# GpSimd's work on the diagonal term, one loop split in two: all r k u products of a group, then its three sums times v

## What is computed

```python
for t in range(S):
    cur = np.einsum('bhd,bhe->bhde', u[None] * kt, vt)
    y[:, :, t] = np.einsum('bhd,bhde->bhe', rt, state + cur)
    state = wt[:, :, :, None] * state + np.einsum('bhd,bhe->bhde', kt, vt)
...
g = np.where(pos, h, np.where(neg, 0.0, (h + beta) ** 2 / (4.0 * beta)))   # h = x @ w_in
x = g @ w_out
...
out = (silu(x @ w_gate) * (x @ w_val)) @ w_out
```

## Time and profile before

| | |
|---|---|
| three runs | 953.28, 955.07, 956.41 us; median 955.07 |
| the profiled execution, its own time | 953.63 us |
| its span, first to last instruction | 951.8 us |
| granted PE clock | 0.999 of full speed |
| busy | PE 98%, DVE 58%, ACT 41%, POOL 18% of the span |

### The profile page before, as it was taken

One profiled execution on the slowest core, in us unless ns is written; L12 is line 12 of the kernel. 1 busy time (PEld: TensorE's weight loads), 2 busy tenths in 40 slices (PEclk: granted clock), 3 DMA queues, 4 the chain that ended last, 5 costly groups with the idle time before them and its releaser, 6 DMA issues.

```text
span 951.8 us, 20721 instructions
## 1 busy us (share of the span) xinstructions
PE 933.3 (98%) x8344; PEld 917.5 (96%) x8344; DVE 548.2 (58%) x975; ACT 392.2 (41%) x827; POOL 173.4 (18%) x155
## 2 busy tenths in 40 slices
PE   6899999999999999999999999999999999999998
PEld 5889999999999999999999999999999999999997
DVE  8998877877777778774444433334343343434333
ACT  5675545455554545535664222222222222222222
POOL 6993220402204022021444100000000000000000
PEclk9999999999999999999999999999999999999999
DMA  9824443344433444212324010010101001010000
GB/s 311 247 83 179 139 135 127 113 148 131 142 123 118 142 134 132 110 58 92 108 84 131 3 51 1 1 51 1 51 0 50 0 0 50 0 50 0 25 1 27
DMA packets 49715, 79.58 MB, mean 84 GB/s; under 512 B 14784, under 2 KB 35648, under 8 KB 49632
## 3 DMA queue, kind: packets, MB, share of 16 engines
q1 hardware_dynamic: 49632, 78.42, 25.2%
HBM read 60.71 MB, written 17.69 MB: 82 GB/s over the span
## 4 chain that ended last, share of the span: by engine, by line
PE 93%; DVE 4%; issue 1%; ACT 0%; DMA 0%; DVEq 0%
PE bank L1438 51%; PE bank L1466 36%; PE bank L1497 2%; PE bank L1528 2%; PE bank L1523 1%; DVE suf L1131 1%; PE bank L1515 1%; DVE k_r_by_channel L1156 0%; DVE k_r_by_channel L1153 0%; DVE att L1198 0%; DVE gate L1280 0%; DVE glo L1273 0%; DMA w_by_channel<-in_w_channel 0%; DVE diag L1161 0%; DVE w_by_channel L1141 0%
## 5 line engine op out<-in xcount | busy, mean ns | idle before, releaser
L970 ACT ACTIVATE ghi<-gate 128x384 fp32r<-128x384 f32 x224 | 117.3, 524 | 207.4 <-DVE gate L1292 95.4
L1273 DVE TENSOR_TENSOR glo<-gate,ghi 128x384 fp32r<-128x384 f32 x224 | 136.6, 610 | 83.6 <-ACT ghi L970 81.8
L1290 DVE TENSOR_TENSOR gate<-bank,gate 128x384 f32<-128x384 f32 x96 | 53.5, 558 | 215.0 <-ACT gate L1091 215.0
L1438 PE MATMUL bank<-xhi,w2gv_ahi 128*128 128x384 f32 x480 | 161.3, 336 | 0.0
L1438 PE MATMUL bank<-xlo,w2gv_ahi 128*128 128x384 f32 x480 | 161.3, 336 | 0.0
L1438 PE MATMUL bank<-xhi,w2gv_alo 128*128 128x384 f32 x480 | 161.3, 336 | 0.0
L1091 ACT ACTIVATE gate<-bank 128x384 f32<-128x384 f32 x96 | 47.2, 492 | 227.7 <-PE bank L1438 227.7
L1466 PE MATMUL bank<-ghi,w1ohi 128*128 128x384 f32 x384 | 132.7, 346 | 0.9 <-DVE glo L1273 0.9
L1438 PE MATMUL bank<-xhi,w1ihi 128*128 128x384 f32 x384 | 129.5, 337 | 1.4 <-issue 0.9
L1438 PE MATMUL bank<-xhi,w1ilo 128*128 128x384 f32 x384 | 129.4, 337 | 0.0
L1466 PE MATMUL bank<-glo,w1ohi 128*128 128x384 f32 x384 | 129.4, 337 | 0.0
(11 more groups left out here) (105 smaller groups left out, 1550.3 us busy)
## 6 DMA issues: line engine op xcount, KB each, us to landing
r_k_v_by_token<-in_rkv_token SPq DMA_DIRECT2D x21, 672.0 KB, 6.1
k_r_by_channel<-in_kr_channel SPq DMA_DIRECT2D x18, 512.0 KB, 4.9
w_by_channel<-in_w_channel SPq DMA_DIRECT2D x24, 226.2 KB, 3.2
k_blocks_out<-k_blocks SPq DMA_DIRECT2D x18, 256.0 KB, 2.1
k_moved<-k_blocks_out SPq DMA_DIRECT2D x72, 64.0 KB, 2.0
x_t<-ring SPq DMA_DIRECT2D x8, 576.0 KB, 3.2
x_raw<-x_t SPq DMA_DIRECT2D x8, 576.0 KB, 4.0
ring<-in_w_out SPq DMA_DIRECT2D x21, 192.0 KB, 2.8
```

The costliest lines, as they stand in the source:

```text
L970: e.activation(ghi[j % 2][:, :], gate[j % 2][:, :], ACT.Copy).then_inc(M["hi", ph], 1)
L1273: e.tensor_tensor(glo[j % 2][:, :], gate[j % 2][:, :], ghi[j % 2][:, :].bitcast(F32), ALU.subtract)\
L1290: e.tensor_tensor(q, hid[j % 2][:, 0:T], q, ALU.mult).then_inc(M["t", 2], 1)
L1438: m = e.matmul(out, w_of(a, k), x_of(b_, k), start=start and i == 0, stop=stop and i == total - 1)
```

## The change

The loop over the windows is run twice for groups 2 to 7: once for the products, and once more for the values. Groups 0 and 1, and all other engines' programs, keep their order; SP's is the same line for line.

```diff
             for g in range(2, NG):
                 for w in range(NW):
                     diag_products(g, w)
+                for w in range(NW):
                     diag_values(g, w)
```

## The result

The changed kernel takes 961.10 us (median of 6 runs, 958.95 to 962.75), the kernel before 955.23 us (6 runs, 953.28 to 956.41). The ratio is 1.0061, 95% interval 1.0047 to 1.0074: 5.9 us slower, 4.5 to 7.1. The forecast was 959.1 us, +4.0.

The account below looks back on a forecast made before the run. PE was taken to bound the kernel; waits of 3.7 us in five groups plus 0.3 in group 0 gave +4.0, 957.6 for the profiled execution, 959.1 as median. Range 957.1 to 962, or 954.3 to 962 including no change.

Parts of the forecast that it names:

- The bound and the question: Whole kernel: PE sets the time, other engines' gains in phase 1 are worth at most 1.9 us; their lead decides losses.
- Where the products land: Group 3's four moved POOL products, 4 us of work, arrive at 262 to 269 us, in slots 11 to 13.
- The walk: Slots 11 to 13: four products successively delay DVE, lo(14) by 2.42 us against a 1.34 us lead; PE waits 1.08 us.
- The rule behind the walk: When POOL and DVE both wait, DVE keeps its turn behind a scan but loses it between ordinary two-operand instructions, costing 0.82 us.
- Step 4: Slot 12, window 2: L851 runs 268.04 to 268.91 us, so L1156 ends at 269.47 instead of 267.05, 2.42 us late.
- The kind of instruction: In slots 11 to 13, two-SBUF-input DVE instructions and SBUF-reading POOL instructions exclude each other; up to 4 us a group.
- the wait of PE: At tile_out(14), PE waits for lo(14): 1.08 us in the walked group, 2.6 us over the other four, together 3.7 us.
- The turn of group 0: Two products land among group 0's scans and delay lo(0) of group 1 by 0.77 us against 0.49 lead; PE waits 0.3.
- The sum: Whole kernel: 3.7 us from five groups plus 0.3 from group 0 gives +4.0 us, 959.1 us after the median adjustment.
- the case of no change: Rival, 33%: DVE keeps its turn in slot 12's scaling, lo(14)'s delay stays under its lead; 955.4 us.
- the added wait bites: Rival, 1%: `tok` lands 15 us later, making the values and L1234 late; five groups at 1 us, 960 us.
- The heavier case: Rival, 6%: every moved product costs DVE the full 0.82 us, adding 9.8 us in all, 964.9 us.

## Why the prediction was right

- *The bound and the question* held: PE sets the time, what DVE won (its wait at L1162) was worth nothing, as the kernel with the later sum shows by itself, and what it lost counted where it passed the lead.
- *Where the products land* held: POOL's first product starts in the scan, its last ends at 272.24 us, slots 11 to 13.
- *The walk* held step by step in group 3: 0.42, 0.35, 0.83 and 0.82 us were forecast for the four records, 0.35, 0.35, 0.82 and 0.82 measured, 2.42 against 2.34 in all. Who went first was as forecast at each of the four steps.
- *The rule behind the walk* is another matter: that DVE keeps its turn behind a scan and loses it between ordinary instructions holds for the pairs that this walk meets, and not in general. The trace of the kernel before had both counterexamples, which the prediction passed over. Behind the scan that ends at 10.29 us POOL's L848, waiting since 9.70, goes first and L1153 takes 1.42 us; behind the ordinary L1156 of the earlier trace rows, which ends at 40.27, DVE's lo goes first with its 0.55 us, though POOL's L851 has waited since 39.80. DVE's timeline, then POOL's:

```profile
9.05 1.24 DVE L1141 TENSOR_TENSOR_SCAN w_by_channel<-w_by_channel,scan_seed 112x516 f32<-112x516 f32 x1
10.20 1.42 DVE L1153 TENSOR_TENSOR k_r_by_channel<-k_r_by_channel,suf 112x512 f32<-112x512 f32 x1
...
40.20 0.55 DVE L1273 TENSOR_TENSOR glo<-gate,ghi 128x384 fp32r<-128x384 f32 x1
...
9.70 1.38 POOL L848 TENSOR_TENSOR r_k_v_by_token<-r_k_v_by_token 128x384 f32<-128x384 f32 x1 [5.04 <-DMA r_k_v_by_token<-in_rkv_token]
...
39.80 1.81 POOL L851 TENSOR_TENSOR r_k_v_by_token<-r_k_v_by_token,u_rows 128x384 f32<-128x384 f32 x1
```

For scan then lo and for L1153 then L1156 the kernel before had rows, and the forecast stood on them; for L1268 then L1153 it had none, and that this pair went the same way was in part luck. Step 4 took place in group 3 alone: elsewhere L1157 was not held up. For the other four groups the prediction shows no steps, so its 2.6 us for them, 3.0 measured, can't be compared step by step.
- *The kind of instruction* held. In the changed kernel, as in the rule of the Trainium skill (SBUF — State Buffer, Who interferes with whom), it is two-input instructions against a reading GpSimd operation; the fills that only write agree with it too, with a 0.53 us lo issued beside one.
- *The term that was too small* is the wait of PE. I took 269.45 us from the chain of waits as the moment when tile_out(14) starts; PE's timeline has its first matmul at 269.29. The lead was 1.18 us, not 1.34, and the tile behind a wait loses another 0.04 to 0.17. That is 0.3 us in group 3 (1.34 for 1.08), and 4.3 us for the five groups in place of 3.7. Single groups were off both ways, group 4 by -0.3, so that the sum is nearer than its parts. The five waits themselves are 0.25 to 1.07 us, where about 1 us each was to be seen. The turn of group 0 cost 0.54 for 0.3: the same reading had made its lead 0.49, and PE's timeline has 98.16 - 97.83 = 0.33.
- *The sum*: +4.0 forecast, 4.9 by the places in the trace, +5.9 (4.5 to 7.1) by the runs. Between the last two the interval decides nothing; I have no further cause to name.
- *The rivals*: the case of no change needed DVE to keep its turn in the scaling, and L1154 with 1.50 us in all five groups says no. That the added wait bites is refuted by the kernel held to lo(15), which has it and the time of before. The heavier case, 964.9, was just not reached even with twice the operations (964.59; its interval reaches 965.9).

What stays open: what decides who goes first when both engines wait, why PE pauses in slot 6 of group 1, and what makes the start differ. That the last two are not the change's is judged from the other kernels, which show them too. No kernel here beats the one before; two that keep the new order (held to lo(15) in groups 3 to 7, or with lo(14) ahead of the scaling) equal it.

## What to carry to other kernels

Moving idle-engine work to an earlier moment is not free because that engine was idle: list which instructions of its neighbour on the shared ports stand at the new moment, and how long a lead the next result behind them has on the bounding engine. The lead is one allowance that several small delays share, so try the parts together, and look at every deadline in the stretch, the copy of an output tile as well as the operand of the next matmul. Read the lead from the bounding engine's timeline, not from the chain of waits, whose pieces began 0.16 us late here. Putting the result that the bounding engine wants ahead of the work that can be delayed gives the lead back.

## What of the hardware was new to me

- When POOL has been waiting for a two-input DVE instruction to end and the next one has been issued too, who goes first depends on the pair, and the same way each time. Counted over the traces of the kernels here except the one with fills: lo went first behind a scan (93 cases, 0.52 to 0.54 us) and behind L1156 (22 cases, 0.54 to 0.55); POOL went first ahead of L1153 behind a scan (16), ahead of L1156 behind L1153 (62), ahead of L1153 behind L1268 (14) and ahead of lo behind L1268 (10), and the DVE instruction then took 1.25 to 1.51 us. What decides it these runs do not show; the kind of the instruction before does not.
- A held-up POOL operation can grow as much as it makes others grow: L851 took 2.33 us at 267.19 in place of 1.01, blocked through a scan and the lo behind it.
- A DVE instruction beside a POOL fill that only writes is not held up (0.53 us, with 0.25 us of overlap), nor is the fill (0.42 us, issued within a scan of 1.23).
- In the kernel with twice the work PE waited 2.01 us to 397.71 us, and in the stretch 399.20 to 402.00 us its granted clock was 0.50; the next tile_out started 1.67 us late. A wait of PE can cost more than itself.
